# The strided heads' values of batches 1 to 3 issued by GpSimd instead of SyncE, in a fused attention, expert and MLP kernel

## What is computed

```python
mask_local = (rel >= 0) & (rel < stride)                     # heads 0 to 3
mask_strided = (rel >= 0) & (pos[None, :] % stride == pos[:, None] % stride)   # heads 4 to 7
attn = np.exp(scores - scores.max(-1)); attn /= attn.sum(-1) + 1e-9
out = np.matmul(attn, v)          # stride 32
```

## Time and profile before

| | |
|---|---|
| time, median of 3 runs | 760.3 us (759.5 to 762.51) |
| the profiled execution's own time | 757.96 us |
| its span, first to last instruction | 755.9 us |
| mean granted TensorE clock | 0.983 |
| PE busy | 712.7 us, 94% of the span |
| DVE, ACT, POOL busy | 279.1, 231.7, 184.3 us |
| DMA queue q1 (hardware, issued by SP) | 60040 packets, 58.60 MB |
| DMA queue q0 (software, issued by POOL) | 7504 packets, 22.44 MB |

### The profile page before, as it was taken

One profiled execution on the slowest core, in us unless ns is written; L12 is line 12 of the kernel. 1 busy time (PEld: TensorE's weight loads), 2 busy tenths in 40 slices (PEclk: granted clock), 3 DMA queues, 4 the chain that ended last, 5 costly groups with the idle time before them and its releaser, 6 DMA issues.

```text
span 755.9 us, 12260 instructions
## 1 busy us (share of the span) xinstructions
PE 712.7 (94%) x4674; PEld 662.7 (88%) x4674; DVE 279.1 (37%) x597; ACT 231.7 (31%) x505; POOL 184.3 (24%) x173
## 2 busy tenths in 40 slices
PE   4999999776998999999999999999999999999997
PEld 3899999666998999998999998999999899999996
DVE  5867778458212111113232223223232322323222
ACT  2667666331111111122232223222232322223222
POOL 5242220104197777761100300210030011001000
PEclk9999999896999999999999999999999999999999
DMA  8484845574788989940100200110020001001001
GB/s 174 107 190 114 230 123 158 171 251 124 275 266 285 307 286 310 316 151 20 42 1 1 84 1 0 43 42 1 0 83 0 0 28 55 0 0 43 1 0 42
DMA packets 68653, 81.76 MB, mean 108 GB/s; under 512 B 26137, under 2 KB 47417, under 8 KB 68602
## 3 DMA queue, kind: packets, MB, share of 16 engines
q1 hardware_dynamic: 60040, 58.60, 26.0%
q0 software_dynamic: 7504, 22.44, 9.3%
q10 hardware_dynamic: 1058, 0.02, 0.1%
HBM read 68.84 MB, written 12.21 MB: 107 GB/s over the span
## 4 chain that ended last, share of the span: by engine, by line
PE 86%; DVE 4%; DMA 3%; ACT 3%; issue 3%; SPq 0%; another core or an unknown queue 0%; POOL 0%; ACTq 0%; POOLq 0%; DVEq 0%
PE psum L1679 26%; PE psum L1696 26%; PE psum L1565 9%; PE psum L1581 8%; PE psum L1443 4%; PE psum L1464 3%; ACT kt L884 2%; PE psum L1415 2%; PE psum L1453 2%; PE psum L1434 1%; PE psum L1598 1%; PE psum L1591 1%; DVE sc L1063 1%; DMA x_sb<-x_rows 1%; DMA x_rows<-xo 1%
## 5 line engine op out<-in xcount | busy, mean ns | idle before, releaser
L1380 DVE SCALAR_TENSOR_TENSOR g_act<-g_raw 128x384 f32<-128x384 f32 x96 | 53.6, 558 | 229.4 <-ACT g_raw L1019 229.4
L1679 PE MATMUL psum<-x2h,wih 128*128 128x384 f32 x384 | 130.7, 340 | 1.5 <-issue 1.5
L1679 PE MATMUL psum<-x2h,wil 128*128 128x384 f32 x384 | 129.4, 337 | 0.0
L1679 PE MATMUL psum<-x2l,wih 128*128 128x384 f32 x384 | 128.9, 336 | 0.0
L1019 ACT ACTIVATE g_raw<-psum 128x384 f32<-128x384 f32 x96 | 47.2, 492 | 235.7 <-PE psum L1679 235.7
L1696 PE MATMUL psum<-woh,g_l 128*128 128x512 f32 x288 | 114.0, 396 | 0.0
L1696 PE MATMUL psum<-wol,g_h 128*128 128x512 f32 x288 | 113.7, 395 | 0.0
L1696 PE MATMUL psum<-woh,g_h 128*128 128x512 f32 x288 | 112.2, 390 | 0.5 <-DVE g_l L1384 0.5
L857 POOL DMA_INDIRECT out_dram<-o_sb,idxo x15 | 16.0, 1067 | 282.7 <-ACT o_sb L1014 279.7
L1565 PE MATMUL psum<-xt,wring 128*128 128x160 f32 x512 | 81.6, 305 | 1.5 <-issue 1.5
L1581 PE MATMUL psum<-hp,wring 128*128 128x160 f32 x512 | 78.4, 299 | 1.3 <-issue 0.7
(11 more groups left out here) (210 smaller groups left out, 869.0 us busy)
## 6 DMA issues: line engine op xcount, KB each, us to landing
wring<-in_moe_w_dram SPq DMA_DIRECT2D x64, 512.0 KB
x_sb<-x_rows SPq DMA_DIRECT2D x4, 1024.0 KB, 6.3
stage<-in_moe_w_in_dram POOLq DMA_DIRECT2D x4, 1024.0 KB
stage<-in_moe_w_out_dram POOLq DMA_DIRECT2D x4, 1024.0 KB
q_st<-in_q_dram SPq DMA_DIRECT2D x7, 576.0 KB
k_st<-in_k_dram SPq DMA_DIRECT2D x7, 576.0 KB
vs<-in_v_dram SPq DMA_DIRECT2D x20, 128.0 KB, 8.2
x_rows<-xo SPq DMA_DIRECT2D x8, 288.0 KB, 7.5
```

Of the source, the lines that this page charges most:

```text
L1380: dve.scalar_tensor_tensor(out=g_act[:, f % 2, :], in0=g_raw[:, f % 2, :], scalar=LEAK, in1=g_raw[:, f % 2, :], op0=ALU.mult, op1=ALU.max) ...
L1679: last = pe.matmul(bank[f % 2][:, 0:MT * P], wt[:, c, f * P:(f + 1) * P], xp[:, T.par, c, :], start=(c == 0 and n == 0), stop=(c == KD - 1 ...
```

## The change

The strided groups' values of batches 1 to 3 (3 batches x 5 groups x 4 heads = 60 DMAs) are issued by GpSimd. It does so after its four copies of batch b: for each strided group g it waits for `s_xo` of (b - 1, g), increments the semaphore `s_tick` (`carry`), and issues the four DMAs. They count on new semaphores `s_vp`, and `values` waits for those from batch 1 on. SyncE still issues the strided values of batch 0 and all local values. The rows, the destination and the sizes of each DMA are as before.

```diff
+        s_vp = {g: sem(f"s_v{g}_by_pool") for g in range(NL, NG)}
...
-        def v_load(eng, b, g):
+        def v_load(eng, b, g, landed=s_v):
...
-                eng.dma_start(vs[0:G["m"], g, h, 0:DH], src).then_inc(s_v[g], 16)
+                eng.dma_start(vs[0:G["m"], g, h, 0:DH], src).then_inc(landed[g], 16)
...
-                    if b + 1 < B:
+                    if b + 1 < B and g < NL:
                         v_load(sp, b + 1, g)
...
                         pool.tensor_copy(to, what).then_inc(s_in, 1)
+                if b:
+                    for g in range(NL, NG):
+                        pool.wait_ge(s_xo, NG * (b - 1) + g + 1)
+                        carry()
+                        v_load(pool, b, g, s_vp)
...
                 pe.wait_ge(s_pte, n + 1)
-                pe.wait_ge(s_v[g], v_count(g) * b + v_count(g))
+                if g < NL or b == 0:
+                    pe.wait_ge(s_v[g], v_count(g) * b + v_count(g))
+                else:
+                    pe.wait_ge(s_vp[g], v_count(g) * b)
```

More of the change, by code:

```diff
@@ L455, in v_load @@
                 src = vb[:, 0:HL, s0:s0 + P - lo, :].rearrange("o h s d -> s (o h) d")
-                eng.dma_start(vs[lo:P, g, :, 0:DH], src).then_inc(s_v[g], 16)
+                eng.dma_start(vs[lo:P, g, :, 0:DH], src).then_inc(landed[g], 16)
                 return
```

## The result

| | before | after |
|---|---|---|
| median | 759.9 us (6 runs, 757.51 to 762.51) | 751.47 us (6 runs, 749.49 to 753.53) |
| profiled execution, its own time | 757.96 us | 753.53 us |
| its span | 755.9 us | 751.5 us |
| POOL busy | 184.3 us | 220.3 us |
| DMA queue q1 (SP) | 60040 packets | 52744 packets |

The ratio is 0.9894, with a 95% interval of 0.987 to 0.9917: a gain of 8.1 us, between 6.3 and 9.9 (the medians differ by 8.4). The direction was right, the size was not: 754.4 us was forecast, and 751.47 lies half a microsecond under the range of 752 to 767.

What follows compares the result with a forecast made beforehand. SP's late issue of strided values was taken to bound the attention's end; -6.8 us there plus a 0.9 us stand gave -5.9 us, from a 760.3 us median to 754.4 us, range 752 to 767.

Steps and rivals of the forecast that it cites:

- What bounds the kernel: End of the attention: SP is behind issuing strided values, 0.75 us per DMA, so TensorE waits 2.03 and 2.32 us.
- Part 1: SP loses 60 issues; gain wholly from the end of the attention onward, 6.8 us, between 6.1 and 7.6.
- 5.4 us for the end of the attention: Values of (3, 9) and (3, 10) come in time; last xo at 134.45 instead of 139.82.
- 0.7 for the clock: Router's first 16 transposes: time lost to the low clock comes back, bounds 0 and 1.5 us, middle taken.
- 0.68 at tile 13: Router: TensorE's stand ahead of tile 13 goes, as the last store issues at 134.5 instead of 141.97.
- c: Time from one strided-value DMA to the next on POOL; taken as 0.84 us, bounds about 0.74 and 1.25.
- the stand of 0.9 us: TensorE at batch 2's first chunk, 63 us, waits for GpSimd's copy of q, delayed behind twenty DMAs.
- POOL gives back what SP gains: Rival: at c = 1.0, stands of 4.1 and 3.05 us, time 760.7; c from 0.90 to 1.09 has chance 0.22.
- POOL becomes the bound: Rival: at c = 1.25, next batch's copy of q is late, time 770.7; c over 1.09 has chance 0.18.
- the formula: TensorE's stands for copies of q: 20c - 15.9 us at batch 2, a further 20c - 16.95 us at batch 3.
- VectorE's hold: Rival: each POOL DMA waits for a VectorE instruction, c would be 1.26, time 771.1; chance 0.04.
- The end does not move: Rival: last values or batch 3's read back come no earlier; at most 2 us gained, about 758.3 to 760; chance 0.06.

Runs made afterwards that it cites:

- two disjoint parts of the change: Against the kernel before, only batch 3's 20 strided-value DMAs moved to GpSimd: 751.54 us, ratio 0.9901; only the 40 of batches 1 and 2: 751.97 us, 0.9902.
- The two comparisons of the whole change: The changed kernel against the kernel before, first 751.47 us, ratio 0.9894, then again unaltered, 751.63 us beside 760.16, ratio 0.9899.
- the three profiles of before: The kernel before, unaltered, profiled three times: 757.96, 765.37 and 758.18 us.
- the third profile of before: The kernel before, unaltered, run once more for another profile: 758.18 us.
- 27 and 31 us for twenty DMAs: Changed kernel with a GpSimd memset behind each of its 60 DMAs, 128 x 320 then 128 x 560: 776.98 us, ratio 1.0243, and 785.03 us, ratio 1.035.

## Why the prediction was right in direction and wrong in size

**What bounds the kernel: right.** SP's issue of strided values was the cause, shown by two disjoint parts of the change that each give all of it, one of them with the last values still on SP.

**Part 1, the sum of 6.8 us: right for the profile that it was made from.** Its terms, 5.4 us for the end of the attention, 0.7 for the clock and 0.68 at tile 13, came out at 5.2 and, together for the router, 1.6 us (router start to the first instruction of VectorE behind it, 24.70 us before and 23.08 after). 5.2 + 1.6 = 6.8.

**The first step that failed is the size of c, and with it the stand of 0.9 us in the sum.** c was taken as 0.84, the duration of the nearest kind of DMA, and is 0.62. The stand that this put ahead of batch 2's first chunk measured nothing. The direct DMA was the right kind to take, but the line through L745 and L803 gave too high a value even as the lower bound, 0.74: the 126 pieces cost less than the line through 512 and 2304 says. With c = 0.62 the forecast would have been 760.3 - 6.8 = 753.5 us, inside the range and still 2 us above the measured median. 0.4 of these 2 us are the median of before, 759.9 and not 760.3.

**The second is the one from that execution to the median, and with it the range.** I took a gain worked out from one execution, bounded it by 6.1 and 7.6 us, and subtracted it from the median. So even without a stand nothing below 752.7 us was foreseen, and the range ended at 752. The two comparisons of the whole change give 8.1 and 7.7 us, its two parts 7.5 each. What the removed stands cost is not the same in each execution. By the same measure, from xo of (0, 6) to the router's start and through the router, the three profiles of before lose 6.8, 17.4 and 6.0 us against the changed kernel. The stand at tile 13, 0.68 us in the first, was 1.86 and 0.17 us in the others, and where it was 1.86 us the clock fell as well and the router took 32.6 us instead of 24.3. The range needed the scatter of the stands themselves.

**Where the missing microsecond comes from stays open.** For more costly stands in the median execution speaks the mean granted clock: 0.983 in the profile that the prediction read, 0.976 to 0.982 in all 54 timed executions of before, with 0.979 as their median, and 0.983 to 0.988 in the 12 of the changed kernel. Against it speaks the third profile of before, which has 0.977, a clock as the timed ones have, and loses only 6.0 us at these stages; the rest of its low clock lies in the index arithmetic and after it, where the change does nothing. The costly one, 17.4 us, is no guide to the median, since no timed execution is like it. And 6.8 us lies within the interval of each comparison, so scatter elsewhere, such as the 2.2 us ahead of the first scores, can be the whole of it.

**The rivals.** "POOL gives back what SP gains" and "POOL becomes the bound" had the right mechanism and place, confirmed at 27 and 31 us for twenty DMAs, with the formula within 1.3 us for the stands. It has no term for the clock behind them, which cost some 9 us more in the first of the two. Their condition was not met. VectorE's hold exists and has nothing to act on here. "The end does not move" was wrong.

## What to carry to other kernels

A queue that issues in order carries its lateness to the end of its stage: look at what the last consumers wait for, and expect the same gain from taking enough work off anywhere ahead of that point, up to the size of the backlog and no further. Where little is taken off, look for waits in the queue itself: here a wait for stores to land took up 2.3 of 5.8 us. When work is moved onto an engine whose other products have a fixed date, write down the room (here 16 us for twenty DMAs) and measure the cadence. A gain worked out from one profile is that execution's. Where what is removed is a short stand of TensorE, take a second profile, since the same stand can also cost the clock, and compare the mean granted clock of the profile with that of the timed executions.

## What the runs showed of the hardware that I had not expected

- A direct DMA by GpSimd of 126 pieces of 256 bytes takes 0.62 us, less than SP's 0.75 us for the same shape, though most of SP's loads of q and k, with 288 pieces, take only 0.4 to 0.6 us.
- A wait of GpSimd for its own memset costs about 0.3 us ahead of a DMA and 0.70 us where a second wait follows. The 60 DMAs without such a wait follow each other with no gap within a group.
- Stands of 1.86 and 2.66 us ahead of tile 13 were followed by 37 us and by ten microseconds at the lower level of the clock (the 37 run on through the index arithmetic); those of 0.17, 0.68 and 1.07 us at the same place by none. The length of a stand does not decide alone: one of 1.13 us ahead of the router's first transposes was followed by 3.4 us at the lower level with batches 1 and 2 on GpSimd, and by none in the changed kernel.
